# Gated attention and two FFN layers on one core: products of zeros in TensorE's waits, other queues for the first loads, a level product moved

## The reference

```python
# q, k, v, f_logit: (4, 8, 768, 48)
f = sigmoid(f_logit)
for t in range(768):
    state = f[:, :, t, :, None] * state + k[:, :, t] (outer) v[:, :, t]
    y[:, :, t] = q[:, :, t] @ state
x = y as (3072, 384)
h = x @ w_in;   g = where(h > 0, h, exp(min(h, 0)) - 1);  x = g @ w_out       # first layer, 384 -> 2048 -> 384
h = relu(x @ w2_in);                                      out = (h * h) @ w2_out  # second layer
```

## Time and profile before

| | |
|---|---|
| median of 3 runs | 1005.48 us (1005.15 to 1005.61) |
| profiled execution | 1005.5 us, span 1003.7 us |
| TensorE busy | 966.9 us, 96% of the span |
| VectorE, ScalarE, GpSimd busy | 534.9, 390.6, 302.3 us |
| first level product starts | 8.48 us |
| TensorE waits within the last column's products of chunk 0 | 49.9 to 51.7 us |
| first FFN product starts | 54.16 us |

### The profile page before, as it was taken

One profiled execution on the slowest core, in us unless ns is written; L12 is line 12 of the kernel. 1 busy time (PEld: TensorE's weight loads), 2 busy tenths in 40 slices (PEclk: granted clock), 3 DMA queues, 4 the chain that ended last, 5 costly groups with the idle time before them and its releaser, 6 DMA issues.

```text
span 1003.7 us, 27605 instructions
## 1 busy us (share of the span) xinstructions
PE 966.9 (96%) x11972; PEld 823.4 (82%) x11972; DVE 534.9 (53%) x758; ACT 390.6 (39%) x685; POOL 302.3 (30%) x243
## 2 busy tenths in 40 slices
PE   5888888999999999999999999999999999999998
PEld 4777766888888888878787879999999999999997
DVE  5679595676767686766425663333333333333332
ACT  3436542434543443443435443232242332322322
POOL 4547573544545363535332542000000000000000
PEclk9989998999999999999999999999999999999999
DMA  8244323221320313022002322000010010000000
GB/s 262 57 138 123 107 65 96 67 64 39 92 77 22 97 35 96 24 56 71 11 2 95 98 83 72 1 32 32 1 63 0 19 44 0 31 31 0 32 1 31
DMA packets 54187, 56.88 MB, mean 57 GB/s; under 512 B 19520, under 2 KB 46400, under 8 KB 54080
## 3 DMA queue, kind: packets, MB, share of 16 engines
q1 hardware_dynamic: 51376, 44.12, 15.3%
q10 hardware_dynamic: 2704, 11.17, 3.1%
HBM read 45.84 MB, written 9.44 MB: 55 GB/s over the span
## 4 chain that ended last, share of the span: by engine, by line
PE 89%; DVE 4%; issue 3%; ACT 2%; DMA 1%; POOL 0%; SPq 0%; DVEq 0%; POOLq 0%; ACTq 0%
PE ps L1531 8%; PE ps L1530 8%; PE ps L1535 8%; PE ps L1569 7%; PE ps L1568 7%; PE ps L1572 7%; PE ps L1068 6%; PE ps L1180 6%; PE ps L1203 5%; PE ps L1182 5%; PE ps L1189 5%; PE ps L1205 5%; PE ps L1209 5%; PE ps L1130 2%; PE ps L1085 1%
## 5 line engine op out<-in xcount | busy, mean ns | idle before, releaser
L1484 DVE TENSOR_TENSOR g<-g 128x512 f32<-128x512 f32 x96 | 66.8, 696 | 263.9 <-ACT g L1404 263.9
L666 POOL TENSOR_TENSOR glo<-g,ghi 128x512 fp32r<-128x512 f32 x80 | 109.5, 1369 | 235.9 <-ACT ghi L489 235.9
L1404 ACT ACTIVATE g<-ps 128x512 f32<-128x512 f32 x112 | 66.9, 598 | 284.7 <-PE ps L1535 280.4
L1530 PE MATMUL ps<-xhi,wts 128*128 128x512 f32 x336 | 131.9, 393 | 0.7 <-ACT xhi L474 0.7
L1531 PE MATMUL ps<-xhi,wts 128*128 128x512 f32 x336 | 131.9, 393 | 0.0
L1569 PE MATMUL ps<-wts,ghi 128*128 128x384 f32 x380 | 128.9, 339 | 0.0
L1568 PE MATMUL ps<-wts,ghi 128*128 128x384 f32 x380 | 127.6, 336 | 0.0
L482 ACT ACTIVATE e<-ps 128x512 f32<-128x512 f32 x80 | 47.7, 596 | 153.3 <-PE ps L1189 153.2
L1180 PE MATMUL ps<-xhi,wts 128*128 128x512 f32 x240 | 99.0, 413 | 2.1 <-ACT g L483 1.3
L1203 PE MATMUL ps<-ghi,wts 128*128 128x512 f32 x234 | 95.8, 409 | 3.4 <-ACT ghi L489 3.4
L873 DVE TENSOR_SCALAR e<-e 128x512 f32<-128x512 f32 x80 | 45.7, 571 | 96.1 <-ACT e L482 95.9
(11 more groups left out here) (118 smaller groups left out, 1664.4 us busy)
## 6 DMA issues: line engine op xcount, KB each, us to landing
raw<-w SPq DMA_DIRECT2D x64, 192.0 KB, 2.4
q<-qk SPq DMA_DIRECT2D x22, 256.0 KB, 4.0
gate<-fl SPq DMA_DIRECT2D x10, 512.0 KB, 5.3
k<-qk SPq DMA_DIRECT2D x10, 512.0 KB, 3.7
x<-xo ACTq DMA_DIRECT2D x6, 768.0 KB, 3.4
xs<-x ACTq DMA_DIRECT2D x6, 768.0 KB, 4.3
out<-PT SPq DMA_DIRECT2D x24, 192.0 KB, 1.9
v<-vn SPq DMA_DIRECT2D x11, 384.0 KB, 3.5
```

The source lines that it names most:

```text
L666: nc.gpsimd.tensor_tensor(out=glo[:, f % 2, :], in0=g[:, f % 2, :], in1=ghi[:, f % 2, :].bitcast(F32), op=ALU.subtract).then_inc(s_glo, 1)
L1530: nc.tensor.matmul(h, w(0, k), xhi[:, k, :], start=(k == 0), stop=False)
```

## The change

- TensorE: `keep_warm(n, banks)` now multiplies zeros of `state` (128 columns of weights, 256 moving columns, fp32) into the half of a bank that the level products do not use. Seven such products stand ahead of the first level product in place of the two of 384 columns. In chunk 0 one stands ahead of each level product from level 1 on and ahead of each unit's key transposes, 14 in all. For this `product` and `transpose_keys` wait for the bank first, then run it, then wait for the q and k updates.
- GpSimd's memset of `state` goes ahead of that of `PT`; the counts waited for follow.
- The second half of unit 0's gates is loaded from ScalarE's queue, second of its loads, and no longer from SyncE's.
- `product(1, 0, 1)` goes between `hidden(1, 0)` and `hidden(1, 1)`; VectorE does `rest(1, 0, 1)` (take and double) ahead of `activate(1, 1)`.

```diff
-        def load_half(c, h, u):
-            sp.dma_start(keys_of(c, h)[:, u * W:(u + 1) * W], ...).then_inc(s_k_in[h % 2], 16)
-            sp.dma_start(gate[:, h % 2, u * W:(u + 1) * W], ...).then_inc(s_f[h % 2], 16)
...
         load_q(0, 0)
-        load_half(0, 0, 1)
+        sp.dma_start(keys_of(0, 0)[:, W:2 * W], qk[1, :, W:2 * W]).then_inc(s_k_in[0], 16)
         load_q(0, 1)
...
         act.dma_start(keys_of(0, 0)[:, 0:W], qk[0, :, W:2 * W]).then_inc(s_k_in[0], 16)
-        act.dma_start(gate[:, 0, 0:W], fl[0, :, :]).then_inc(s_f[0], 16)
+        for u in range(UB):
+            act.dma_start(gate[:, 0, u * W:(u + 1) * W], fl[u, :, :]).then_inc(s_f[0], 16)
...
         nc.gpsimd.memset(queries(0, 0)[:, :, 0:1], 0.0).then_inc(s_zero, 1)
+        nc.gpsimd.memset(state[:, :, :], 0.0).then_inc(s_zero, 1)
         nc.gpsimd.memset(PT[:, :, 0:2 * X, :], 0.0).then_inc(s_zero, 1)
-        nc.gpsimd.memset(state[:, :, :], 0.0).then_inc(s_zero, 1)
...
             q_update(1, 0, 1)
+            rest(1, 0, 1)
             activate(1, 1)
-            rest(1, 0, 1)
             split_weights(split_at(1, 1))
...
+        def keep_warm(n, banks):
+            for _ in range(n):
+                nc.tensor.matmul(banks[:, 0, 256:512], state[:, 1, 0:P], state[:, 0, 0:256], start=True, stop=True)
...
-            else:
-                pe.wait_ge(*level(s_q, c, h, l - 1))
-                pe.wait_ge(*level(s_k, c, h, l - 1))
             if not past(c, h, 2):
                 if l < 2:
                     pe.wait_ge(s_psum, 2 * l + h + 1)
                 elif l < LEVELS - 1:
                     pe.wait_ge(*taken(c, h, l - 1))
                 else:
                     pe.wait_ge(s_ev4, count(c, h, 1, 1))
+                if l:
+                    keep_warm(1, level_pair(c, h, l))
+            if l:
+                pe.wait_ge(*level(s_q, c, h, l - 1))
+                pe.wait_ge(*level(s_k, c, h, l - 1))
...
         def transpose_keys(c, h):
-            pe.wait_ge(*level(s_k, c, h, LEVELS - 1))
             if not past(c, h, 2):
                 pe.wait_ge(s_ident, 16)
                 pe.wait_ge(s_ev5, count(c, h, 2, 2))
+                keep_warm(1, pair(c, h, "A"))
+            pe.wait_ge(*level(s_k, c, h, LEVELS - 1))
...
-            feed(1, 0, (1, 3))
+            feed(1, 0, (1,))
             product(1, 0, 1)
+            feed(1, 0, (3,))
             feed(1, 0, (4, 5))
...
-        keep_warm(2)
-        pe.wait_ge(s_zero, 1)
+        pe.wait_ge(s_zero, 2)
+        keep_warm(7, pair(0, 0, "Y"))
```

More of the change, by code:

```diff
@@ L313, in load_padded_v @@
                 sp.dma_start(to[:, :, 4 * P - D:4 * P], at[:, :, DM - D:DM]).then_inc(s_vz[h % 2], 16)
-        def load_half(c, h, u):
-            sp.dma_start(keys_of(c, h)[:, u * W:(u + 1) * W], qk[c * B + 2 * h + u, :, W:2 * W]).then_inc(s_k_in[h % 2], 16)
-            sp.dma_start(gate[:, h % 2, u * W:(u + 1) * W], fl[c * B + 2 * h + u, :, :]).then_inc(s_f[h % 2], 16)
         def load_weights(chunks):
@@ L415, in take4 @@
             act.wait_ge(*taken(c, h, EARLY))
-            act.wait_ge(s_zero, 2)
+            act.wait_ge(s_zero, 3)
             data = level_pair(c, h, 4)[:, :, 0:X * 32].rearrange("p j (x t) -> p j x t", x=X)
@@ L820, in take @@
                 dve.wait_ge(s_mask, 2)
-                dve.wait_ge(s_zero, 2)
+                dve.wait_ge(s_zero, 3)
             w = 1 << l
@@ L834, in state_update @@
             else:
-                dve.wait_ge(s_zero, 3)
+                dve.wait_ge(s_zero, 2)
             for j in range(2):
@@ L1034, in product @@
                     pe.wait_ge(s_ev4, count(c, h, 1, 1))
-            elif not past(c, h, 3):
+                if l:
[3 more added lines that the diff above has]
+                pe.wait_ge(*level(s_k, c, h, l - 1))
+            if past(c, h, 2) and not past(c, h, 3):
                 if l == 0:
@@ L1041, in product @@
                     pe.wait_ge(*taken(c, h, l - 1))
-            elif l in (1, 2):
+            elif past(c, h, 3) and l in (1, 2):
                 pe.wait_ge(*taken(c, h, l))
-            elif l == 3:
+            elif past(c, h, 3) and l == 3:
                 pe.wait_ge(s_ev6, count(c, h, 1, 0))
-            elif l == 4:
+            elif past(c, h, 3) and l == 4:
                 pe.wait_ge(*taken(c, h, EARLY))
@@ L1077, in transpose_keys @@
                 pe.wait_ge(s_ev5, count(c, h, 2, 2))
-            elif more(c, h):
+                keep_warm(1, pair(c, h, "A"))
+            pe.wait_ge(*level(s_k, c, h, LEVELS - 1))
+            if past(c, h, 2) and more(c, h):
                 pe.wait_ge(*taken(c, h + 1, EARLY - 1))
-            else:
+            elif past(c, h, 2):
                 pe.wait_ge(s_ys, count(c, h, 1, -2))
@@ L1286, in second_period @@
             end_of_y(1, 1)
-        def keep_warm(n):
-            for _ in range(n):
-                nc.tensor.matmul(ps[:, PAIR_Y, 0:DM], e[:, 0, 0:P], e[:, 0, 0:DM], start=True, stop=True)
         pe.wait_ge(s_warm, 1)
         pe.wait_ge(s_psum, 1)
-        keep_warm(2)
-        pe.wait_ge(s_zero, 1)
+        pe.wait_ge(s_zero, 2)
+        keep_warm(7, pair(0, 0, "Y"))
         for l in range(LEVELS):
```

## The result

The changed kernel takes 1011.63 us (median of 5 runs, 1011.16 to 1014.0); the kernel before, run beside it, 1005.61 us. The ratio is 1.0062 (95% interval 1.0046 to 1.0077): slower by 0.6%. Forecast was 1002.4 us.

What follows compares the result with a forecast made beforehand. The prediction took TensorE's FFN stream to bound the kernel from about 115 us, VectorE and GpSimd the early levels; terms 0 - 2.7 + 0 - 0.2 - 0.2 = -3.1 gave 1005.5 - 3.1 = 1002.4 us, range 999.8 to 1007.5.

Steps and rivals of the forecast that it cites:

- hidden: Chunk 0 levels: single zero products lie in TensorE's idle time, 3.0 us a level against VectorE's 2.8 to 5.2; 0 lost.
- rival A: Levels of chunk 0: zeros do not hold the clock; up to 6.2 us lost, put at +3, 1008.5; chance 0.20.
- The size of a single: Each of the fourteen single zero products: 0.43 us at the upper clock, 0.85 at the lower.
- halved case: Levels of chunk 0: the clock rises late, so about half of up to 6.2 us counts: +3, 1008.5 us.
- The gain of a high clock: Levels, transposes and first values products: level 3 -0.7, last updates and transposes -1.6, values -0.4; sum -2.7 us.
- the predicted tail: Last updates and key transposes of units 0 and 1: faster at the high clock, together -1.6 us.
- The prediction's sum by that rule: Clock gain if the full clock does not engage for transposes: the 1.6 us goes, leaving -1.1 us.
- The loads: Start: unit 1's gates and the mask 1.0 us later, against shorter VectorE operations; 0, ends -0.8 and +1.2 us.
- The level product's move: Between hidden(1, 0) and hidden(1, 1): the level product fits TensorE's 1.27 us wait; -0.2 us, ends -1.1 and +1.0.
- ScalarE's exponential of tile 2: After the moved level product: this exponential starts 0.5 us later, VectorE's q update of level 2 0.2 us sooner.
- The fall of the clock near 51 us: After the transposes: the clock falls again behind the untouched wait, stream arrives earlier; -0.2 us, ends -2.4 and 0.
- rival C: Last column's products, near 50 us: the clock holds through them too, -5.3 us, 1000.2 us; chance 0.12.

Runs made afterwards that it cites:

- gap filled: Changed kernel, its 14 single products kept, with eight more products of zeros between the level-0 products of units 0 and 1: ratio 1.0055, 1011.0 us.

## Why the prediction was wrong

**The step that failed** is the word "hidden" under the fourteen single products of zeros: that with the level product at about 1.1 us a pair of units costs TensorE 3.0 us a level, against 2.8 to 5.2 us of VectorE. That holds only at the upper clock. The prediction had the clock rise with the seven products and fall again in the wait for unit 1's queries, and for its coming up once more it had one reason, given against rival A: that TensorE busy without a gap is "what preceded both rises". The rise was right (1.12 us for the first level product), and so, but for a microsecond, was the fall. The second rise did not come: from 13.5 to 47.6 us TensorE was busy without a gap and the clock stayed down. At level 3 a pair of units took TensorE 5.6 us (25.64 to 31.24), two singles at 1.15 and two level products at 1.65, instead of 3.0, and VectorE waited. That is rival A, given 0.20, with the very sign that the prediction named for it.

Gapless work was the wrong reading of what had preceded the rises. What had preceded the rise at 57.6 us was dense 512-column work, while small products nearly without a gap had not raised it; zeros among small products, 15.9 us of 33, did not change that. With the clock given as a present (gap filled) it fell again, and only two products a place held it.

**The size of a single** was put at 0.85 us at the lower clock, from columns alone. It is 1.15 from its start to the level product behind it. From the level-1 product of unit 0 to the transposes the changed kernel takes 31.55 us (14.63 to 46.18). Twelve of the fourteen singles lie in it, eleven at 1.15 us and the last at 1.02: 13.7 us, which leaves 17.9 us of level products. Before, the same stretch was 24.5 us, so 6.6 us of waits had been there to hide them in, and 13.7 do not go into 6.6: +7. Of that about 1 us came back at the load of queries, and the end moved by 6.1.

Rival A came to "up to 6.2 us" by luck: three errors nearly cancelled (0.85 us a piece for 1.15, fourteen pieces where twelve stood in the way, 5.8 us of idle time for 6.6), and the microsecond that came back was not foreseen. I then halved it to +3, for a clock that would rise late; it rose only when the transposes had begun. The range's upper end, 1007.5, lay below even the halved case's own 1008.5, so it did not take in "the greater part of A", as the prediction says, and the measured 1011.63 lies outside.

**The gain of a high clock**, -2.7, was never seen by itself. Where the clock was high for all levels it had been bought with zeros. There the stretch from unit 1's level-6 product to the end of the transposes is 4.4 us against 5.0, with 1.8 us of zeros in it (from their starts to those of the transposes behind them), so something like the predicted tail is real; what it would be without its price, no run here shows.

**The transposes** run faster at the high clock (272 ns against 421, 1.04 us a unit), as the rows of before had it. The Trainium skill ("TensorE: Matmul & The Clock Gate", Part 4: PE-mode transpose) has the full clock not engage for them; the runs with a high clock disagree (eight instructions in 1.04 us against 1.91). The prediction's sum by that rule, -1.1, also took away the 0.2 us of a level product; it should have been -1.3.

**The loads**: the sum 0 was right, its parts too large. The mask was 0.3 to 0.5 us later, not 1.0, and the doubling beside GpSimd was indeed shorter (0.72 us) in the changed kernel. With the loads alone it still took 1.37 us, so the loads did not bring this by themselves.

**The level product's move**: 0 measured for -0.2 predicted. The prediction's 0.5 us for "ScalarE's exponential of tile 2" was not what took it: it came 0.4 us later after the relu (9.21 us for 8.85), but VectorE reached that activation later still, at 71.30. In the profile it was GpSimd's update, which came to lie beside another VectorE instruction.

**The fall of the clock near 51 us** came again behind the same wait, which now lies from 55.4 to 57.3 us; the fall is at 57.8. This speaks against rival C. (By windows of 0.1 us the changes of the clock in the kernel before lie at 50.8, 57.6 and 129.3 us, 0.1 us sooner than the prediction has them, and the changed kernel's at 13.5 and 47.6, where the expectations say 13.7 and 47.7; nothing rests on the difference.)

## What to carry to other kernels

Work that is put into waits is free only as long as it is shorter than the wait in the state of the clock that it really runs in: count the waits (here 6.6 us), multiply the filler by its measured distance to the next instruction (1.15 us, not its 0.85 us of columns), and do it for the lower clock first. Before buying a high clock, ask what waits for TensorE: here VectorE and GpSimd set the pace, and neither a high first level nor the loss of all zeros changed the time. And when moving a piece saves time at one point, look at the next point of the same kind: an overlap of GpSimd and VectorE moved along with it and took the time back.

## What the runs showed of the hardware

- The column of the granted clock starts with the first recorded change. The kernel with the singles alone shows 1.00 for 60 us with level products as slow as those at 0.50.
- Products of nothing but zeros can bring the upper clock. In all six profiles of kernels with seven of 256 columns at the start the first level product took 1.12 us. With two of 384 columns it took 1.93 us in four profiles and 1.60 in one, and without any 1.94.
- TensorE busy without a gap from 14 to 47 us, on one zero product and one level product (64 or 32 small instructions on 48 rows) in turn, stayed at 1.2 GHz. With two zero products in turn with the level product, entered at 2.4 GHz, it stayed there, though waits of over 1 us lay between.
- A full-array fp32 product of 256 columns ahead of small ones costs 1.15 us at the lower clock and 0.6 at the upper (14.09 to 14.71 us with the gap filled), one of 64 columns 0.61 at the lower.
